# Expert weights fetched in eight transfers of 512 KB instead of four of 1 MB, and the first result rows scaled on VectorE instead of GpSimd

## The reference

```python
def _moe2_ref(x, w_gate, w_noise, noise, w1, w2):      # x: 2304 x 512, E = 8, F = 1024
    logits = x @ w_gate
    noisy_logits = logits + np.log1p(np.exp(x @ w_noise)) * noise
    top2 = np.argpartition(-noisy_logits, 2, axis=1)[:, :2]
    ...                                                  # top2_w: softmax over the two
    for e in range(E):
        for k in range(2):
            mask = top2[:, k] == e
            h = np.maximum(x[mask] @ w1[e], 0.0)         # w1[e]: 512 x 1024
            out[mask] += top2_w[mask, k, None] * (h @ w2[e])   # w2[e]: 1024 x 512
```

## Time and profile before

| | us |
|---|---|
| median of three runs (1019.12 to 1026.11) | 1021.15 |
| the profiled execution | 1021.77 |
| its span | 1020.1 |
| TensorE matmuls busy in it | 985.9 (97%) |
| GpSimd busy in it | 504.7 (49%) |
| VectorE busy in it | 439.2 (43%) |
| mean granted TensorE clock | 0.993 of full |

### The profile page before, as it was taken

How to read it: one execution, slowest core, us unless ns; L and a number is a source line. 1 busy time by engine, 2 the same in 40 slices (tenths; PEclk the granted TensorE clock), 3 DMA queues, 4 the chain that set the end, 5 groups by cost and what they waited for, 6 DMA issues and landing times.

```text
span 1020.1 us, 18598 instructions
## 1 busy us (share of the span) xinstructions
PE 985.9 (97%) x5883; PEld 834.0 (82%) x5884; DVE 439.2 (43%) x830; ACT 340.9 (33%) x483; POOL 504.7 (49%) x761
## 2 busy tenths in 40 slices
PE   6999999999999999999999999999999999999993
PEld 6888988988988988988878878778787878888882
DVE  5453355344345345464555443334343344343114
ACT  2333333332343343332423333333333333333331
POOL 5994001101100200597563867848485785914694
PEclk9999999999999999999999999999999999999997
DMA  8822032132132120624365665646566564338429
GB/s 325 320 89 63 21 105 87 44 119 85 42 84 103 63 63 2 226 84 164 123 227 137 167 173 134 174 123 175 164 172 167 142 167 129 87 92 204 128 76 336
DMA packets 119836, 137.39 MB, mean 135 GB/s; under 512 B 80352, under 2 KB 80480, under 8 KB 119776
## 3 DMA queue, kind: packets, MB, share of 16 engines
q1 hardware_dynamic: 95536, 70.79, 24.2%
q0 software_dynamic: 12288, 44.05, 13.7%
q10 hardware_dynamic: 11952, 21.76, 7.0%
HBM read 77.07 MB, written 40.63 MB: 115 GB/s over the span
## 4 chain that ended last, share of the span: by engine, by line
PE 61%; POOL 25%; DMA 6%; issue 4%; DVE 2%; POOLq 1%; ACT 1%; ACTq 0%; DVEq 0%; SPq 0%
PE ps L1232 20%; PE ps L1246 13%; POOL W L490 11%; PE ps L1219 8%; POOL W L486 8%; PE ps L1351 7%; PE ps L1250 6%; DMA y_lo<-routed_y,y_rows 4%; POOL y_lo L544 3%; POOL y_hi L527 2%; PE ps L1268 1%; PE ps L1188 1%; POOL EXraw L473 1%; PE ps L1167 1%; POOLq L465 1%
## 5 line engine op out<-in xcount | busy, mean ns | idle before, releaser
L1219 PE MATMUL ps<-W,xg_part 128*128 (+1 forms) x1032 | 249.2, 396 | 5.0 <-POOLq L497 4.2
L1351 PE MATMUL ps<-W,hT_part 128*128 (+1 forms) x1032 | 251.1, 398 | 1.2 <-ACT hT_part L740 1.2
L1219 PEld LDWEIGHTS ps<-W,xg_part 128*128 128x128 f32 x1032 | 192.6, 187 | 53.6 <-issue 7.4
L1232 PE MATMUL ps<-x_part,W 128*128 128x384 f32 x1152 | 224.9, 344 | 2.7 <-issue 2.1
L1351 PEld LDWEIGHTS ps<-W,hT_part 128*128 128x128 f32 x1032 | 191.2, 189 | 43.4 <-issue 1.7
L1232 PEld LDWEIGHTS ps<-x_part,W 128*128 128x128 f32 x1152 | 200.9, 189 | 7.9 <-issue 3.2
L449 POOL DMA_INDIRECT routed_x<-x,slot_blk x36 | 36.5, 1014 | 320.5 <-DVE slot_blk L883 224.9
L490 POOL TENSOR_TENSOR W<-EXraw,W 128x256 fp32r<-128x256 f32 x224 | 165.0, 770 | 4.7
L1246 PE MATMUL ps<-W,g_part 128*128 128x512 f32 x576 | 149.9, 395 | 0.0
L486 POOL TENSOR_SCALAR W<-EXraw 128x256 fp32r<-128x256 f32 x224 | 106.5, 504 | 80.4 <-PE ps L1351 72.7
L1246 PEld LDWEIGHTS ps<-W,g_part 128*128 128x128 f32 x576 | 106.9, 188 | 17.7
(11 more groups left out here) (183 smaller groups left out, 811.6 us busy)
## 6 DMA issues: line engine op xcount, KB each, us to landing
EXraw<-in_w POOLq DMA_DIRECT2D x24, 1024.0 KB, 6.0
QKV<-qkv SPq DMA_DIRECT2D x15, 768.0 KB, 5.4
routed_y<-y_sb ACTq DMA_DIRECT2D x43, 256.0 KB, 3.9
routed_y<-zero_tile SPq DMA_DIRECT2D x14, 768.0 KB, 7.3
xg<-routed_x ACTq DMA_DIRECT2D x40, 256.0 KB, 2.9
Wraw<-w_moe SPq DMA_DIRECT2D x16, 512.0 KB, 8.9
EXraw<-in_w SPq DMA_DIRECT2D x8, 1024.0 KB, 7.5
out<-y_lo SPq DMA_DIRECT2D x18, 256.0 KB, 4.8
```

The source lines that it names most:

```text
L1219: last = nc.tensor.matmul(dst, a(ha), b(hb), start=(i == 0), stop=(i == n - 1))
L1232: last = nc.tensor.matmul(ps[:, f % 2, 0:TOK], W[hw][:, f * PIECE + n * P:f * PIECE + (n + 1) * P], x_part[par][hx][:, n, :], start=(n == ...
L1351: last = nc.tensor.matmul(ps[:, 4, :], hT_part[hh][:, n, :], W[hw][:, weights(slot, W1W + n * DM, DM)], start=(n == 0 and k == 0), stop=(n ...
```

## The change: what it does

Two edits. The transfers that GpSimd issues for the next expert's weights are half as large and twice as many: eight of 512 KB, one after each part of 1024 columns, with eight semaphores in place of four. And the 18 multiplications of `y_lo` move from GpSimd, where they stood between the two gathers, to VectorE, where they stand behind its last expert tile (`take_y(GL - 1)`) and ahead of the sums of line 1154.

```diff
--- before.py
+++ after.py
@@ -264,7 +264,7 @@
         hT_in_psum = sem("hT_in_psum")
         hh_ready = sem("hh_ready")
         hl_ready = sem("hl_ready")
-        ex_fetched = [sem(f"ex_fetched{c}") for c in range(4)]
+        ex_fetched = [sem(f"ex_fetched{c}") for c in range(8)]
         up_first = sem("up_first")
         halves_ready = [sem(f"halves_ready{s}") for s in range(2)]
         halves_turned = [sem(f"halves_turned{s}") for s in range(2)]
@@ -463,12 +463,12 @@
             def load_expert(p, c):
 
                 e = pool.value_load(order_tab[0:1, p:p + 1], min_val=0, max_val=E - 1)
-                raw = EXraw[:, c * WQ:(c + 1) * WQ]
-                if c < 2:
-                    src = w1v[e, :, 2 * c:2 * c + 2, :]
+                raw = EXraw[:, c * SUB:(c + 1) * SUB]
+                if c < 4:
+                    src = w1v[e, :, c:c + 1, :]
                     dst = raw.rearrange("p (n f) -> p n f", f=F2)
                 else:
-                    src = w2v[e, :, 4 * (c - 2):4 * (c - 1), :]
+                    src = w2v[e, :, 2 * (c - 4):2 * (c - 3), :]
                     dst = raw.rearrange("p (n f) -> p n f", f=DM)
                 nc.gpsimd.dma_start(dst, src).then_inc(ex_fetched[c], 16)
 
@@ -477,8 +477,8 @@
                     at_w = (p % 2) * SLOT
                     if c % 2 == 0 and p == 1:
                         pool.wait_ge(ex_loaded[c // 2], 32)
-                    elif c % 2 == 0:
-                        pool.wait_ge(ex_fetched[c // 2], 16 * (p - 1))
+                    elif p > 1:
+                        pool.wait_ge(ex_fetched[c], 16 * (p - 1))
                     if p == 1:
                         pool.wait_ge(g2_done, NF * (NB - 1) + NF // 2 + c + 1)
                     for part in narrow(c * SUB):
@@ -489,9 +489,9 @@
                         piece = slice(at_w + part.start, at_w + part.stop)
                         nc.gpsimd.tensor_tensor(W[LO][:, piece], EXraw[:, part], W[HI][:, piece].bitcast(F32),
                                                 ALU.subtract).then_inc(ex_taken, 1)
-                    if c % 2 == 1 and p + 1 < E:
+                    if p + 1 < E:
                         pool.wait_ge(ex_taken, SUB // NARROW * (8 * (p - 1) + c + 1))
-                        load_expert(p + 1, c // 2)
+                        load_expert(p + 1, c)
                 if parts[-1] == 7:
                     pool.wait_ge(ex_taken, SUB // NARROW * 8 * p)
                     pool.sem_inc(ex_ready, 1)
@@ -537,12 +537,6 @@
                 if t >= ABREAST:
                     pool.wait_ge(lo_got[t % ABREAST], 16 * (t // ABREAST))
                 gather(t, 0, y_lo[t][:, :], lo_got[t % ABREAST])
-            pool.wait_ge(wmix_ready, 2)
-            for r in range(ABREAST):
-                pool.wait_ge(lo_got[r], 16 * T // ABREAST)
-            for t in range(T):
-                nc.gpsimd.tensor_scalar(y_lo[t][:], y_lo[t][:], wmix[:, t, 0:1], None, ALU.mult).then_inc(lo_scaled, 1)
-
             done = pool.value_load(done_tab[0:1, E - 1:E], min_val=1, max_val=G)
             pool.wait_ge(y_stored, done * 16)
             pool.sem_inc(wait_carrier, 1)
@@ -1148,6 +1142,11 @@
             take_y(GL - 1)
 
 
+            dve.wait_ge(wmix_ready, 2)
+            for r in range(ABREAST):
+                dve.wait_ge(lo_got[r], 16 * T // ABREAST)
+            for t in range(T):
+                nc.vector.tensor_scalar(y_lo[t][:], y_lo[t][:], wmix[:, t, 0:1], None, ALU.mult).then_inc(lo_scaled, 1)
             for t in range(T):
                 dve.wait_ge(lo_scaled, t + 1)
                 dve.wait_ge(hi_got[t], 16)
```

## The result

| | before | after |
|---|---|---|
| median, us (four runs each) | 1020.35 | 1074.06 |
| profiled execution, us | 1021.77 | 1073.36 |
| its span, us | 1020.1 | 1071.7 |
| TensorE's waits for the split weights (line 497), us | 4.2 | 51.6 |
| mean granted TensorE clock | 0.993 | 0.969 |

The changed kernel takes 1.0515 times as long, 95% interval 1.048 to 1.0551.

The account below looks back on a forecast made before the run. GpSimd's split and TensorE, nearly balanced, form the bounding 59.1 us cycle. Span 1020.1 + 55.5 (experts) - 9 (tail) = 1066.6, plus 1.7 outside it: 1068.3 us; forecast 1053 to 1080 (0.64), whole range 1048 to 1086.

Parts of the forecast that it names:

- The issues: GpSimd's splits of p = 2 to 6: four more issues each at 2.0 us, 40 us in all, bounds 29 and 59.
- p = 1: Split of expert 1: added issues in its second half release TensorE 1.5 to 3.3 us late, taken as 2.
- The clock: TensorE's first product after five longer waits runs at a lowered clock: 2.5 us each, 12.5 in all.
- The tail: After the last expert: gathers no longer wait for GpSimd's multiplications, TensorE's last store ends the span; -9 us, bounds -8 and -11.
- rival of the starved gathers: Tail: VectorE's multiplications hold up the first `y_hi` gather, losing 6.5 of the 9 us: 1075 us; chance 0.10.
- The rival on the other side: Not slower: an issue's price goes with its bytes, the cycle stays at 59.1 us, only the tail counts: 1013 us; chance 0.05.

Follow-up runs that it names:

- filled kernel with 16 matmuls: Changed kernel plus 16 small matmuls of unused result per tile, ahead of TensorE's wait for the weights: 1068.61 us, ratio 1.0447.
- lagged kernels: Each issue one part later: on the changed kernel (eight transfers) 1008.68 us, 0.9871; on the kernel with only the multiplications moved (four) 1010.78 us, 0.9869.
- two kernels with 2 MB transfers: Two transfers per expert, against the kernel with only the multiplications moved: 1012.49 us; the same with each multiplication just ahead of its sum: 1011.85 us.

## Why the prediction was right

The forecast was 1068.3 us; 1074.1 were measured. The mechanism was the forecast one: stops on GpSimd's path, longer waits of TensorE, a lowered clock behind them, a shorter tail. By its own steps:

- **The issues.** 2.0 us each were taken. In the trace an added issue costs 1.8 to 2.0: the stop stayed (1.28 us on average against 1.22), and the DMA instruction shrank from 0.75 to 0.6 (w1) and from 0.80 to 0.77 (w2). The 20 added issues come to 38.5 us, close to the 40. What the term lacked is the other 8.2 us of the splits' 46.7, GpSimd's own instructions that met VectorE's more often; it had no term for them. The bounds, 29 and 59, held the sum. One reading was wrong: that the DMA instruction hardly depends on the number of pieces. At equal bytes it took 0.6 us with one piece per partition (w1) and 0.77 with two (w2), while two pieces of twice the bytes took 0.75.
- **p = 1.** 2 us and 1 us for the clock were forecast; the start of the next split moved by 1.3 and the clock did not fall, after a wait of 0.74 us.
- **The clock.** 12.5 us forecast, 10.6 measured, in five slow products of 1.3 to 2.6 us each. The filled kernel with 16 matmuls shows that it is the standing still that does it.
- **The tail.** -9 was forecast and -9.6 came, but in a different way. TensorE's last store was taken to end the span alone, with the gathers 2 us ahead of it. In fact the first gather was held up for 4 us by VectorE's multiplications, the mechanism of the rival of the starved gathers, at half its price since a multiplication takes 0.40 us and not 0.69. The two paths came out level. The Trainium skill's page "SBUF — State Buffer", section "Who interferes with whom", says that VectorE and GpSimd share a pair of ports as an exclusive lock, which a tensor_scalar on VectorE can take. The trace agrees: the issue took 5.07 us among the multiplications and 0.95 without.
- **Not in the sum.** 2.6 us in the last tiles: 1.6 of them the last product at the lower clock, behind a wait of 1.25 us that the kernel before had too without a fall. No run ties this to the change: over the 13 profiled executions of all kernels here this product took 5.8 to 5.9 us in five and 7.1 to 8.5 in eight.
- **Luck.** In span the terms missed by +6.7 (splits), +2.6 (last tiles), -1.9 (clock), -1.7 (p = 1) and -0.6 us (tail). They cancel in part, to +5.1; the tail's term was right in size through a path that was not foreseen.
- **The rival on the other side** needed an added issue to cost under 0.45 us. In the changed kernel it costs 1.8 at least. The lagged kernels show where that rival would have been right: with the stop hidden, eight transfers and four give the same ratio (0.9871 and 0.9869).

## What to carry to other kernels

Where an engine both computes on the critical path and issues transfers, price an issue by the stop around it, not by its bytes: here 1.2 us in which the engine waits for its own last instruction and its queue then loads a register and comes to the DMA instruction, then 0.6 to 0.8 us. Issue for data that was finished one step earlier, and the wait and the load hide behind the engine's own work; here four or eight transfers then made no difference. Two engines that are balanced to 1 us have no room for such a stop, and a wait that grows from 1 to 10 us on TensorE costs twice, once as a wait and once as clock.

## What the runs showed of the hardware that I had not expected

- The DMA instruction on GpSimd took 0.58 to 0.60 us for 128 x 1024 and 0.76 to 0.78 for 128 x 2 x 512 (512 KB each), 0.75 for 128 x 2 x 1024 and 0.80 for 128 x 4 x 512 (1 MB each).
- A multiplication of 128 x 512 float32 by a value per partition took 0.40 us on VectorE (7.21 for 18) and 1.56 on GpSimd, and a gather that GpSimd began among those 18 on VectorE was held until they were over: it took 5.07 us and ended 0.8 us behind the last.
- TensorE's clock fell after two of four waits between 1.79 and 1.86 us in one kernel, and neither after one of 2.66 us there nor after waits of 2.0 us in another; it fell after waits of 3.4 and 2.7 us in the two kernels with 2 MB transfers. What decides between them stays open.
